# A hashed-attention and two-MoE kernel: pairs 1 to 7 hashed inside pair 0, bucket numbers through HBM, first split on three engines

## What is computed

```python
q_bits = (np.einsum('bhsd,dk->bhsk', q, proj) > 0).astype(np.int64)
k_bits = (np.einsum('bhsd,dk->bhsk', k, proj) > 0).astype(np.int64)
q_bucket = np.sum(q_bits * powers, axis=-1)      # powers = 2 ** arange(6)
k_bucket = np.sum(k_bits * powers, axis=-1)
mask = q_bucket[:, :, :, None] == k_bucket[:, :, None, :]
scores = np.where(mask, scale * np.matmul(q, k.transpose(0, 1, 3, 2)), -1000000000.0)
scores = scores - np.max(scores, axis=-1, keepdims=True)
attn = np.exp(scores)
attn = attn / (np.sum(attn, axis=-1, keepdims=True) + 1e-09)
out = np.matmul(attn, v)
```

## Time and profile before

| | us |
|---|---|
| median of 3 runs | 730.69 (730.4 to 732.74) |
| profiled execution, its own time | 731.03 |
| its span on the core | 729.2 |
| attention, from the start to the last product of L1373, about | 256 |
| pair period in the steady loop | 28.33 |

### The profile page before, as it was taken

The page is one execution under the profiler, slowest core; times in us unless marked ns, Lnnn a source line. Parts: engine busy times, 40 slices in busy tenths (PEclk is TensorE's granted clock), DMA queues, the critical chain, the costliest instruction groups (busy, mean ns, idle before and its releaser), DMA issues.

```text
span 729.2 us, 12070 instructions
## 1 busy us (share of the span) xinstructions
PE 704.5 (97%) x3810; PEld 587.8 (81%) x3810; DVE 428.0 (59%) x825; ACT 321.6 (44%) x634; POOL 266.8 (37%) x271
## 2 busy tenths in 40 slices
PE   7799999999999999999999999999999899999994
PEld 3389999999999987888888888888885688877883
DVE  0589999999999956548555643564197611333110
ACT  0078878788787854221222221123144223443221
POOL 0666777677667751007004500720001222121111
PEclk9989999999999999999999999999999999999999
DMA  9921321321233030001100300001135541001011
GB/s 296 264 59 55 105 55 55 97 65 54 80 81 117 1 116 0 1 2 58 58 1 0 115 0 0 1 8 51 58 132 183 190 161 59 29 30 45 32 56 47
DMA packets 22508, 51.32 MB, mean 70 GB/s; under 512 B 3168, under 2 KB 5344, under 8 KB 22464
## 3 DMA queue, kind: packets, MB, share of 16 engines
q1 hardware_dynamic: 19008, 42.34, 18.3%
q0 software_dynamic: 2480, 7.87, 3.3%
q10 hardware_dynamic: 976, 0.56, 0.3%
HBM read 44.47 MB, written 6.55 MB: 70 GB/s over the span
## 4 chain that ended last, share of the span: by engine, by line
PE 89%; DVE 4%; DMA 2%; ACT 1%; issue 1%; SPq 1%; ACTq 0%; POOL 0%; POOLq 0%; DVEq 0%
PE ps L1373 9%; PE ps L1392 9%; PE ps L1576 6%; PE ps L1578 6%; PE ps L1577 6%; PE ps L1540 6%; PE ps L1542 6%; PE ps L1541 6%; PE ps L1406 5%; PE ps L1407 5%; PE ps L1661 3%; PE ps L1663 3%; PE ps L1662 3%; PE ps L1631 3%; PE ps L1633 3%; PE ps L1632 3%
## 5 line engine op out<-in xcount | busy, mean ns | idle before, releaser
L678 ACT ACTIVATE pt_hi<-ps 128x384 fp32r<-128x384 f32 x192 | 88.0, 499 | 42.1 <-PE ps L1392 26.9
L939 DVE TENSOR_TENSOR pt_lo<-ps,pt_hi 128x384 fp32r<-128x384 f32 x192 | 100.1, 551 | 10.4 <-ACT pt_hi L678 6.3
L731 ACT ACTIVATE relu<-ps 128x512 f32<-128x512 f32 x48 | 28.7, 598 | 175.6 <-PE ps L1542 175.6
L667 ACT ACTIVATE probs<-ps,neg_max 128x768 f32<-128x768 f32 x96 | 87.3, 909 | 26.0 <-DVE neg_max L930 25.9
L1392 PE MATMUL ps<-cst,probs 128*128 128x128 f32 x576 | 90.7, 275 | 0.9 <-DVE pt_lo L939 0.9
L930 DVE TENSOR_REDUCE neg_max<-ps 128x1 f32<-128x768 f32 x96 | 90.9, 946 | 0.0
L1117 DVE TENSOR_TENSOR sq<-relu 128x512 f32<-128x512 f32 x48 | 36.4, 759 | 71.6 <-ACT relu L731 71.2
L1540 PE MATMUL ps<-xt_hi,wi_hi 128*128 128x512 f32 x192 | 75.8, 395 | 0.0
L1576 PE MATMUL ps<-wo_hi,g_hi 128*128 128x512 f32 x192 | 74.9, 390 | 0.6 <-DVE xt_lo L1007 0.6
L1392 PEld LDWEIGHTS ps<-cst,probs 128*128 128x128 f32 x576 | 70.6, 145 | 5.9 <-DVE pt_lo L939 1.6
L1542 PE MATMUL ps<-xt_hi,wi_lo 128*128 128x512 f32 x192 | 74.8, 390 | 0.0
(11 more groups left out here) (198 smaller groups left out, 1473.0 us busy)
## 6 DMA issues: line engine op xcount, KB each, us to landing
w_raw<-w SPq DMA_DIRECT2D x16, 512.0 KB, 6.8
raw_k<-kT SPq DMA_DIRECT2D x32, 192.0 KB, 3.3
raw_q<-qT SPq DMA_DIRECT2D x32, 192.0 KB, 3.6
wi_raw<-w_in SPq DMA_DIRECT2D x4, 1024.0 KB, 5.1
wo_raw<-w_out SPq DMA_DIRECT2D x4, 1024.0 KB, 5.1
pair_raw<-qT SPq DMA_DIRECT2D x8, 384.0 KB, 6.7
pair_raw<-kT SPq DMA_DIRECT2D x8, 384.0 KB, 13.6
raw_v<-v SPq DMA_DIRECT2D x16, 192.0 KB, 2.4
```

The costliest lines, as they stand in the source:

```text
L939: nc.vector.tensor_tensor(pt_lo[c % 2][sl], unit(tt, h).rearrange("p (k q) -> p k q", k=3), pt_hi[c % 2][sl].bitcast(F32), ALU.subtract).t ...
```

## The change

1. **Head.** Only pair 0 is projected at the start, k before q, with a weight of 12 columns (`projb` is 128 x 12 now). Its bits are 12 x 768, the pattern products (`first_dots`) take 768 columns. VectorE makes the two k masks, ScalarE the two q masks by ReLU(dot + 1 - bit count).
2. **First split on three engines.** q and k of pair 0 reach SBUF by `load_pairs` for one half of the partitions and `load_half` for the other. ScalarE makes five of the copies, VectorE the first `kb` subtraction, GpSimd `q_scaled`, the first `qa` subtraction and the rest of head 1 (`split_first`, `rest_qk`).
3. **Pairs 1 to 7 inside pair 0.** With score tile j + 1 TensorE also projects pair j (`project`): 12 products, each a 128 x 128 f32 block of `pair_raw` as weight and 12 moving columns. VectorE weighs the bits by powers of two, adds them up to bucket numbers and rounds them to bf16 (`make_ids`). With score tile j + 3 TensorE turns them (`turn_ids`), and VectorE keeps 24 x 128 numbers (`keep_ids`).
4. **Through HBM.** SP stores the numbers of pair j (6 KB) to `buckets` and loads a pair's numbers broadcast over 64 partitions, one load a head (`bucket_of`, 128 x 1536 bf16).
5. **Two comparisons a pair.** `next_masks` compares `bucket_of` with the partition's number, once for q, once for k (768 bf16 elements each), at iteration 7 of pair 0 and iteration 3 of the pairs 1 to 6. The 42 mask products and 42 comparisons of before are gone from the pair loops.
6. **Constants.** Two of the loads on ScalarE's queue are issued at the start, five behind the q masks and ahead of the first exponential (`late_in`).

The core of the diff; `sem` lines, buffers and GpSimd's counts are left out:

```diff
-            sp.dma_start(projb[:, :, :], proj_blocks).then_inc(projb_in, 16)
-            for n in range(PIECES):
-                load_pairs(0, n)
+            for c in (1, 0):
+                load_pairs(c, 0)
+
+            load_half(0)
+            load_half(1)
+            for n in range(1, PIECES):
+                for c in (1, 0):
+                    load_pairs(c, n)
+                if n <= 2:
+                    load_v(0, n - 1, True)
+
+            sp.wait_ge(first_qa, 2)
+            sp.wait_ge(first_kb, 1)
+            load_head(1, 0)
+            load_v(1, 0, False)
+            store_ids(1)
+            sp.wait_ge(ids_out, 16)
+            load_buckets(1)
+            sp.wait_ge(qk_split, 6)
+            load_head(1, 1)
+            load_v(1, 1, False)
+            for j in range(2, PAIRS):
+                store_ids(j)
+            sp.wait_ge(ids_out, 16 * (PAIRS - 1))
+            with sp.Fori(2, PAIRS) as i:
+
+                sp.wait_ge(masks_staged, i * 2 - 2)
+                load_buckets(i)
+                for z in range(2):
+
+                    sp.wait_ge(qk_split, i * 12 + (6 * z - 12))
+                    load_head(i, z)
+                    load_v(i, z, False)
 
...
+            act.dma_start(projb[:, :], proj_blocks[:, 0, 0:2 * NBITS]).then_inc(projb_in, 16)
+            for dst, src in ((patt[:, :], patterns[0:2 * NBITS, 0:P]), (cst[:, :], consts)):
+                act.dma_start(dst, src).then_inc(const_in, 16)
+
+            def copied(dst, src, scale):
+                nc.scalar.activation(dst, src, ACT.Copy, scale=scale).then_inc(first_split, 1)
+
+            m, n = half(0, True), half(0, False)
+            act.wait_ge(pairs_in[PIECES], 16)
+            copied(ka[0][m, :], pair_raw[m, 1, 0, :], 1.0)
             act.wait_ge(pairs_in[0], 16)
-            for dst, src in ((cst[:, :], consts), (patt[:, :], patterns), (tri_sb[:, :], tri), (sb_sb[:, :], sb_rows),
-                             (wg_sb[:, :, :], w_gate), (mid_sb[:, :, :], mod_id), (mb_sb[:, :, :], mod_bias)):
-                act.dma_start(dst, src).then_inc(const_in, 16)
+            copied(qa[0][m, :], pair_raw[m, 0, 0, :], SCALE)
+            act.wait_ge(raw_in[0], 32)
+            copied(ka[0][n, :], raw_k[0][n, :], 1.0)
+            copied(qb[0][n, :], raw_q[0][n, :], SCALE)
+            copied(ka[1][half(1, True), :], pair_raw[half(1, True), 1, 0, :], 1.0)
+            act.wait_ge(const_in, 32)
+            act.wait_ge(dots_done, 2)
+            act.wait_ge(popc_known, 1)
+            for z in range(2):
+                part = half(z, True)
+                nc.scalar.activation(qb[z][part, :], dots(0)[part, :], ACT.Relu,
+                                     bias=popc_1[part, 0:1]).then_inc(q_masked, 1)
+            for dst, src in ((tri_sb[:, :], tri), (sb_sb[:, :], sb_rows), (wg_sb[:, :, :], w_gate),
+                             (mid_sb[:, :, :], mod_id), (mb_sb[:, :, :], mod_bias)):
+                act.dma_start(dst, src).then_inc(late_in, 16)
...
+            def make_ids(j, side):
+
+                v_.wait_ge(powers_set, NBITS)
+                nc.vector.scalar_tensor_tensor(
+                    weighed[j % 2][:, :, :], beside(side, 2 * QT * 2 * NBITS).rearrange("p (g b) -> p g b", b=NBITS), 0.0,
+                    powers[:, :].unsqueeze(1).to_broadcast([P, 2 * QT * 2, NBITS]), ALU.is_gt, ALU.mult).then_inc(bits_weighed, 1)
+                v_.wait_ge(bits_weighed, j)
+                nc.vector.tensor_reduce(ids_f[:, :].rearrange("p (z c) -> p c z", z=2),
+                                        weighed[j % 2][:, :, :].rearrange("p (c z) b -> p c z b", z=2), AX,
+                                        ALU.add).then_inc(ids_summed, 1)
+                v_.wait_ge(ids_summed, j)
+                nc.vector.tensor_copy(ids[j % 2][:, :], ids_f[:, :]).then_inc(ids_made, 1)
+
+            def keep_ids(j, side):
+
+                nc.vector.tensor_copy(ids_row[:, j, :], turned_ids(side)).then_inc(ids_kept, 1)
+
+            def next_masks(i):
+
+                v_.wait_ge(ids_in, i * 32 + 32)
+                if not isinstance(i, int):
+                    v_.wait_ge(masks_in, i * 4)
+                v_.wait_ge(lane_known, 1)
+                nc.vector.tensor_scalar(mask_st[:, 0, :], bucket_of[:, 0, :], lane[:, :], None,
+                                        ALU.is_equal).then_inc(masks_staged, 1)
+                nc.vector.tensor_scalar(mask_st[:, 1, :], bucket_of[:, 1, :], lane[:, :], -BIG, ALU.not_equal,
+                                        ALU.mult).then_inc(masks_staged, 1)
 
...
+                if first and 0 < tt - PROJ_TILE < PAIRS:
+                    make_ids(tt - PROJ_TILE, z)
+                if first and 0 < tt - TURN_TILE < PAIRS:
+                    keep_ids(tt - TURN_TILE, z)
...
+                    if tt == (FIRST_MASK_TILE if first else MASK_TILE) and not last_:
+                        next_masks(i)
...
+            def first_dots(c):
+                pe.wait_ge(const_in, 32)
+                pe.wait_ge(bits_done, 2 - c)
+                for lo, hi in ((0, 512), (512, SEQ)):
+                    last_mm = mm(dots(c)[:, lo:hi], patt[:, :], bits[:, c, lo:hi], start=True, stop=True)
+                last_mm.then_inc(dots_done, 1)
-            for c in range(2):
-                for j in range(PAIRS):
-                    if j % PIECE == 0:
-                        pe.wait_ge(pairs_in[PIECES * c + j // PIECE], 16)
-                    if c == 1 and j == 2:
-                        first_masks(0)
-                    for lo, hi in ((0, 512), (512, SEQ)):
-                        last_mm = mm(banks[0:NH * NBITS, 1024 * c + lo:1024 * c + hi], projb[:, j, :],
-                                     pair_raw[:, c, j, lo:hi], start=(j == 0), stop=(j == PAIRS - 1))
+            for c in (1, 0):
+                pe.wait_ge(pairs_in[PIECES * c], 16)
+                for lo, hi in ((0, 512), (512, SEQ)):
+                    last_mm = mm(banks[0:2 * NBITS, 1024 * c + lo:1024 * c + hi], projb[:, :],
+                                 pair_raw[:, c, 0, lo:hi], start=True, stop=True)
                 last_mm.then_inc(proj_done, 1)
-            first_masks(1)
+            for c in (1, 0):
+                first_dots(c)
+
+            def project(j, side):
+
+                for c in range(2):
+                    pe.wait_ge(pairs_in[PIECES * c + j], 16)
+                    for t in range(QT):
+                        at = 2 * NBITS * (QT * c + t)
+                        last_mm = mm(beside(side, 2 * QT * 2 * NBITS)[:, at:at + 2 * NBITS],
+                                     pair_raw[:, c, j, P * t:P * t + P], projb[:, :], start=True, stop=True)
+                return last_mm
+
+            def turn_ids(j, side):
+
+                pe.wait_ge(ident_made, 1)
+                pe.wait_ge(ids_made, j)
+                return nc.tensor.transpose(turned_ids(side), ids[j % 2][:, :], ident_b[:, :])
...
-                if tt in MASK_TILES and not last:
-                    last_mm = masks(i + 1, MASK_TILES.index(tt), beside(tt % 2, MASK_W))
+                if first and 0 < tt - PROJ_TILE < PAIRS:
+                    last_mm = project(tt - PROJ_TILE, tt % 2)
+                if first and 0 < tt - TURN_TILE < PAIRS:
+                    last_mm = turn_ids(tt - TURN_TILE, tt % 2)
```

GpSimd's part for pair 0 (`split_first`):

```diff
+            def split_first():
+                m, n = half(0, True), half(0, False)
+                pool.wait_ge(raw_in[0], 32)
+                copied(q_scaled[n, :], raw_q[0][n, :], SCALE, first_qa, 1)
+                pool.wait_ge(first_split, 4)
+                hold()
+                G.tensor_tensor(qa[0][n, :], q_scaled[n, :], qb[0][n, :].bitcast(F32),
+                                ALU.subtract).then_inc(first_qa, 1)
+                pool.wait_ge(first_qa, 2)
+                m, n = half(1, True), half(1, False)
+                pool.wait_ge(pairs_in[0], 16)
+                pool.wait_ge(raw_in[1], 32)
+                copied(qa[1][m, :], pair_raw[m, 0, 0, :], SCALE, qk_split, 1)
+                copied(ka[1][n, :], raw_k[1][n, :], 1.0, qk_split, 2)
+                rest_qk(1, n, 2)
```

More of the change, by code:

```diff
@@ L1357, in turn_back, with scores @@
                 return last_mm
-            def scores(i, tt, first, last):
+            def scores(i, tt, first):
                 z, j = divmod(tt, QT)
```

208 lines of the change are left out of this document (116 added, 92 removed).

## The result

The changed kernel takes 743.96 us (median of 4 runs, 741.26 to 747.11); beside it the kernel before took 731.07. The ratio is 1.016, 95% interval 1.013 to 1.020: it is slower, where the prediction said 723.6. The profiled execution took 741.26, its span is 739.4.

What follows compares the result with a forecast made beforehand. TensorE, busy 97% of the span, was taken to bound the kernel. From 731.03 us, 3.3 came off for pair 1 opening earlier and 4.1 for mask products in pairs 1 to 6: 723.6, range 721.5 to 726 (55%).

Steps and rivals of the forecast that it cites:

- the clock of pair 0: Pair 0: half pace after TensorE's idle time in the head costs 2.0 us on top of 41.4, so 43.4.
- rival 4: Pair 0: TensorE stays at 1.2 GHz until the last projection block, 28 us more, 751.6 in all; 8%.
- T0: Start of the third score tile, opening pair 0's tile loop; forecast to move from 36.71 to 17.4 us.
- The block, 2.55: Pair 0: each projection block is 24 passes of 0.106 us, 2.55 us, so 17.8 for seven.
- Rival 1: Projection blocks in pair 0: tiny passes run at the transposes' 0.083 us, giving 3.8 us back, 719.8; 9%.
- The head, 17.4: Head: projecting only pair 0 brings the third score tile to 17.4 us, 19.3 earlier; bounds 16.5 and 19.5.
- VectorE's branch: Head: kb subtract, k masks, small operations and neg_max run from 10.9 to 15.0 us, before ScalarE is free.
- Rival 2: Head: third score tile at 19.5 us and 3 us more of half clock, 727.2 in all; 13%.
- The trip through HBM: Pair 1's ids in SBUF at 31.7 us, comparable by 40.5, wanted near 50.5: cover 10 us, costs nothing.
- rival 5: Ids, store, load or placing come over 2 us late and pair 1 waits: 726 to 733; 5%.
- Pairs 1 to 6, 4.1 gained: Steady pairs: 36 mask products removed at 0.115 us each gain 4.1 us; the added comparisons cost nothing.
- Rival 3: Steady pairs: both comparisons wait behind GpSimd instructions, TensorE loses about 0.8 us in seven pairs, 729.2; 9%.

Runs made afterwards that it cites:

- the full fillers: Changed kernel with 120 moving columns, comparisons apart, and TensorE's head idle time filled by 128-row f32 products (2 and 1): 726.51 us median, ratio 0.992 to the kernel before.
- the best version: Changed kernel with 120 moving columns in each block product and the two comparisons in different iterations, no filling products: 726.64 us median, ratio 0.994 to the kernel before.

## Why the prediction was wrong

**The step that failed is the clock of pair 0**, rival 4, which had 8%. The forecast took 41.4 us at full pace and 2.0 for half clock. Measured: 59.4, 16.0 above 43.4. The run with 120 columns splits it. At full clock the pair takes 44.1 (its comparisons stand apart, 0.13 a steady pair; with the full fillers it was 44.15), so 2.7 are work under-sized and 15.3 are half clock, where 2.0 had been put. The rival itself was priced with all blocks at half pace (751.6); the clock oscillated, and about half of that came: 741 to 744.

**The argument against the rival** was the logits and turns at a clock of 1.00. That row is 3.2 us long and holds about 2.3 us of thin passes, in three pieces of under 0.9 with transposes between them; pair 0 has seven blocks of 2.8. A row of a short episode said nothing on the same form repeated for 40 us. The row that spoke for it, 0.50 from 34.00 to 40.60, was put down to the thin stretch and idle time ahead of T0, and priced as an episode of the head. Here TensorE shows no idle time in pair 0.

The Trainium skill ("TensorE: Matmul & The Clock Gate", Part 1: The HAM clock gate) says that activity of the array releases the throttle. The busy column can't be read for that: in pair 0 TensorE shows 59.39 of 59.39 busy at 0.71. The same page of the Trainium skill (HAM oscillation) has such an oscillation from waits for DMA; here it came with no idle time shown.

**The block, 2.55.** Measured 2.76 from start to start at full clock (25.91 to 28.67 with 120 columns), 0.115 a pass against 0.106 of the logits: 1.5 us in seven. Most of the rest of the 2.7 lies in the turns of the ids (0.15 each, not 0.09) and in iteration 7, which took 2.44 instead of 2.15 (2.06 and a turn). The bounds of the forecast (2.0, and half clock) held it. Rival 1, cheaper projections, falls: no pass was under 0.11. The 25 ns that the Trainium skill ("TensorE: Matmul & The Clock Gate", Back-to-back issue gap) gives for the shortest spacing is no price for these products, each with a new weight in f32; the section itself says that this figure leaves the weight load out.

**The head, 17.4.** Right at 16.91, within its bounds, but not by its steps. The first product came at 4.10 (4.7). What ended last was not ScalarE with its DMA issues. Timelines of TensorE, of GpSimd, and of ScalarE with its queue:

```profile
13.13 0.97 PE L1513 MATMUL ps<-ka,qa 128*128 128x512 f32 x2 [2.13 <-POOL qa L587]
```

```profile
9.56 0.83 POOL L578 TENSOR_SCALAR q_scaled<-raw_q 64x768 f32<-64x768 f32 x1 [9.15 <-DMA raw_q<-qT]
11.06 1.98 POOL L587 TENSOR_TENSOR qa<-q_scaled,qb 64x768 fp32r<-64x768 f32 x1 [0.67 <-ACT qb L735]
```

```profile
11.72 0.33 ACTq L755 DMA_DIRECT2D tri_sb<-tri  x1
...
12.59 0.90 ACT L751 ACTIVATE qb<-ps,popc 64x768 fp32r<-64x768 f32 x1
...
13.53 0.45 ACTq L755 DMA_DIRECT2D mb_sb<-mod_bias  x1
15.77 0.90 ACT L766 ACTIVATE probs<-ps,neg_max 128x768 f32<-128x768 f32 x1 [2.29 <-DVE neg_max L1045]
```

The five issues, 11.72 to 13.98, ran beside the second activation and were over 1.8 us before exp 0 could start: they cost nothing, where 2.97 us had been put in the path. Without them the forecast would have had exp 0 at 15.0, behind VectorE's branch. In their place stood what it had called covered: the raw halves came at 9.3 to 9.6 us and not at 6.5, so GpSimd's subtraction ended at 13.04, not 10.1, and held the first scores. These ran at half pace, and VectorE's branch had no term for them: `neg_max` began at 14.78, exp 0 at 15.77. So 1.2 us too much and 0.8 too little, and that 17.4 was near is in part luck. Rival 2, a late head, did not come; its other half, a longer half clock, came through rival 4.

**The trip through HBM** was right in the main. The ids of pair 1 were stored at 34.00 (forecast 31.7; the low clock made it later), the loads issued at 35.33 and landed 3.6 us later, within the bounds of 2.4 and 4.3; the store, 1.3 us until the loads could be issued, was under its bound. The comparisons came at 65. No wait of TensorE in pair 0 is put down to masks, so rival 5 falls. VectorE's id work was 1.0 us a tile, as estimated (0.31 + 0.30 + 0.18 + 0.20), and hidden.

**Pairs 1 to 6, 4.1 gained.** Measured 1.6. The term 0.115 for each of six products was mis-sized: three cost 0.13 and three nothing, 0.40 a pair. The pair of comparisons, called hidden (0.4 in all; they took 0.82), gave back 0.13 on average. 0.40 - 0.13 = 0.27.

**Rival 3**, a comparison held by GpSimd: no comparison was, 0.41 us each, and the cost of the pair came from their own length. But one cast of the ids in pair 0 was long, 1.71 us instead of 0.18, and ended with a subtraction of GpSimd, 47.10 to 48.93. VectorE's timeline:

```profile
47.25 1.71 DVE L1014 CAST ids<-ids_f 128x24 bf16<-128x24 f32 x1
```

That agrees with the rule of the Trainium skill ("SBUF — State Buffer", Who interferes with whom) that the second of the two waits in full. TensorE was in a block then and had no idle time, so it cost nothing. In the run with one product in place of twelve that cover is gone. There a cast of 1.50 us, which also ends with a subtraction of GpSimd, is followed by the longest of TensorE's waits for `pt_lo`, 0.96 us (timeline of all engines):

```profile
33.86 1.83 POOL L602 TENSOR_TENSOR qa<-q_scaled,qb 64x768 fp32r<-64x768 f32 x1 [0.18 <-POOL q_scaled L578]
...
34.23 1.50 DVE L1014 CAST ids<-ids_f 128x24 bf16<-128x24 f32 x1
...
37.23 0.55 PE L1532 MATMUL ps<-cst,probs 128*128 128x128 f32 x3 [0.96 <-DVE pt_lo L1054]
```

So a wait as in rival 3 occurs, at another instruction, and costs something only where TensorE has no block to work on.

Had the clock held, the forecast would have been near: pair 1 opens at 61.18 with 120 columns, against 60.8, and with 2.4 gained in the six pairs that gives 731.03 - 2.9 - 2.4 = 725.7; that execution took 725.85.

## What to carry to other kernels

Read the granted clock beside the busy time. A stretch with seven blocks of f32 products, 128-column weights and 12 moving columns, ran at 1.2 GHz for more than half of its length with TensorE shown busy throughout, and the dense work between the blocks ran at that pace too. Where the weight load sets the pace anyway, a wider moving operand costs next to nothing and can pay: going from 12 to 120 columns took pair 0 from 59.4 to 44.1 us, which no busy share suggests. A term such as "n instructions of 0.12 us each" should be checked for each place: an instruction taken from a TensorE that shows no idle time can still have been hidden.

## What was unexpected in the hardware

- Pair 0 by moving columns, clock and length, one profiled execution each: 12: 0.71, 59.4 us; 36: 0.72, 58.9; 60: 0.91 and 0.90, 48.0 and 48.6; 120: 1.00, 44.1. In the old kernel 12: 0.69, 59.8; 60: 0.93, 45.6.
- 60 or 120 moving columns of f32 stream almost fully beside the weight loads: a block at a clock of 1.00 takes 2.78 and 2.83 us, with 12 columns 2.74.
- Fillers of 12 rows (bf16) did not hold the clock in the two executions profiled (0.50 from 11 to 19 us); fillers of 128 rows (f32) did in the one profiled. Rows, type and number differ between them, so which of these matters isn't shown.
- The granted clock reads 1.00 from 0 to 9 us while the first products ran at half pace (8 instructions in 5.30 us from 4.10, two projections where the earlier trace rows has 1.3 us for one at the full clock), as in the kernel before.
- Two executions of the same program, at a mean clock of 0.995 and 0.985, lie 5 us apart, as much as the best version gains.
